# Moving four small SBUF tiles in the allocation order of a fused two-layer feed-forward kernel, and dropping a spare one

## What is computed

```python
# x [2, 4096, 192], weight_gen [2, 4096, 8, 7]; all arrays float32
w = softmax(weight_gen, axis=-1)                       # 7 taps for each of 8 heads
x = einsum('bshk,bskhg->bshg', w, windows_of_7(x))     # causal, zero-padded
g, val = x @ w_gate, x @ w_val                         # 192 -> 1536
x = (g * sigmoid(g) * val) @ w_out                     # 1536 -> 192
h = x @ w_in                                           # 192 -> 2048
out = (h * clip(h + 3, 0, 6) / 6) @ w_out2             # 2048 -> 192
```

## The kernel before

| tensors | bytes each | first start | remainder by 2048 |
|---|---|---|---|
| all weights, `stage`, `taps` | 3072 to 14336 | 16512 | 128, and for `stage1`, `stage3` 1152 |
| `window` | 7680 | 149760 | 256 |
| `sum_even`, `sum_odd`, `prod_even`, `prod_odd` | 3072 | 157440 | 1792, 768, 1792, 768 |
| `conv_main`, `conv_tail` | 2048, 1024 | 169728 | 1792, 1792 |
| `out_tail` | 1024 | 172800 | 768 |
| `half_col`, `warm`, `spare` | 4, 4, 320 | 173824 | 1792, 1824, 1856 |
| `in1_*`, `in2_*` (eight) | 2048 | 174208 | 128 |
| `mid_main`, `mid_tail`, `swapped` | 2048 | 190592 | 128 |
| `hidden`, `hid_hi`, `hid_lo` | 4096, 8192, 8192 | 196736 | 128 |
| `out_main`, `out_other` | 2048, 1024 | 217216 | 128 |
| `out_rows`, `ident` | 3072, 512 | 220288 | 1152, 128 |

## Time and profile before

### The profile page before, as it was taken

One profiled execution on the slowest core, in us unless ns is written; L12 is line 12 of the kernel. 1 busy time (PEld: TensorE's weight loads), 2 busy tenths in 40 slices (PEclk: granted clock), 3 DMA queues, 4 the chain that ended last, 5 costly groups with the idle time before them and its releaser, 6 DMA issues.

```text
span 1269.5 us, 26488 instructions
## 1 busy us (share of the span) xinstructions
PE 1220.7 (96%) x10696; PEld 1032.1 (81%) x10696; DVE 881.0 (69%) x1353; ACT 650.9 (51%) x1178; POOL 57.6 (5%) x43
## 2 busy tenths in 40 slices
PE   5779999999999999999999999999999999999998
PEld 4557888888898888888888888888889888888876
DVE  7688676676867768686776867667686766864554
ACT  1554654546455453645546464554645545364554
POOL 6441100000000000000000000000000000000000
PEclk9899999999999999999999999999999999999999
DMA  5330001001010100101000010100101010000000
GB/s 163 87 112 23 11 1 44 2 1 44 1 45 1 39 7 1 45 1 44 1 22 24 1 44 2 44 1 7 39 2 44 1 44 2 1 13 1 14 13 14
DMA packets 11766, 32.00 MB, mean 25 GB/s; under 512 B 1048, under 2 KB 5784, under 8 KB 11544
## 3 DMA queue, kind: packets, MB, share of 16 engines
q1 hardware_dynamic: 11672, 30.53, 7.4%
HBM read 24.24 MB, written 6.29 MB: 24 GB/s over the span
## 4 chain that ended last, share of the span: by engine, by line
PE 70%; DVE 13%; ACT 11%; issue 3%; DMA 1%; POOL 0%; ACTq 0%; SPq 0%; POOLq 0%
PE up_bank L787 27%; PE acc L802 16%; PE up_bank L793 14%; PE acc L809 11%; DVE hid_lo L672 6%; DVE hidden L667 5%; ACT hidden L431 5%; DVE in_tail_lo L686 2%; ACT hid_hi L438 1%; PE up_bank L1024 1%; ACT in_tail_hi L453 1%; DMA stage<-in_moe_w_gate_dram 1%; DMA stage<-in_moe_w_val_dram 1%; ACT in_hi L450 1%; ACT swapped L461 1%
## 5 line engine op out<-in xcount | busy, mean ns | idle before, releaser
L787 PE MATMUL up_bank<-in_hi,up_hi 64*128 64x512 f32 x1280 | 350.7, 395 | 18.0 <-DVE hidden L664 12.3
L809 PE MATMUL acc<-hid_hi,dn_tail 64*128 64x512 f32 x872 | 342.4, 393 | 11.6 <-DVE hid_lo L672 10.7
L787 PE MATMUL up_bank<-in_hi,up_lo 64*128 64x512 f32 x1280 | 346.2, 388 | 0.0
L787 PE MATMUL up_bank<-in_lo,up_hi 64*128 64x512 f32 x1280 | 345.9, 388 | 0.0
L802 PE MATMUL acc<-hid_hi,dn_hi 64*128 64x512 f32 x872 | 342.3, 393 | 0.0
L802 PE MATMUL acc<-hid_lo,dn_hi 64*128 64x512 f32 x872 | 337.4, 387 | 0.0
L802 PE MATMUL acc<-hid_hi,dn_lo 64*128 64x512 f32 x872 | 337.3, 387 | 0.0
L809 PE MATMUL acc<-hid_lo,dn_tail 64*128 64x512 f32 x872 | 337.3, 387 | 0.0
L667 DVE SCALAR_TENSOR_TENSOR hidden<-hidden,up_bank 128x512 f32<-128x512 f32 x256 | 176.1, 688 | 209.7 <-ACT hidden L431 208.5
L672 DVE TENSOR_TENSOR hid_lo<-hidden,hid_hi 128x512 fp32r<-128x512 f32 x448 | 313.0, 699 | 1.0
L431 ACT ACTIVATE hidden<-up_bank,half_col 128x512 f32<-128x512 f32 x256 | 176.4, 690 | 242.0 <-DVE hid_lo L672 129.7
(11 more groups left out here) (87 smaller groups left out, 1400.1 us busy)
## 6 DMA issues: line engine op xcount, KB each, us to landing
window<-in_x_dram SPq DMA_DIRECT2D x14, 960.0 KB
out_dram<-out_rows SPq DMA_DIRECT2D x16, 384.0 KB, 2.3
stage<-in_moe_w_out_dram SPq DMA_DIRECT2D x7, 384.0 KB, 3.5
window<-in_x_dram SPq DMA_DIRECT2D x4, 472.5 KB
taps<-in_weight_gen_dram SPq DMA_DIRECT2D x1, 1568.0 KB, 13.0
stage<-in_moe_w_in_dram SPq DMA_DIRECT2D x4, 256.0 KB, 2.7
stage<-in_moe_w_gate_dram SPq DMA_DIRECT2D x3, 256.0 KB, 2.7
stage<-in_moe_w_val_dram SPq DMA_DIRECT2D x3, 256.0 KB, 8.3
```

The costliest lines, as they stand in the source:

```text
L787: return nc.tensor.matmul(dst[:, :], w[lane[half], col:col + P], a[lane[half], :], start=first and product == 0, stop=False)
L809: return nc.tensor.matmul(acc[y][1], dn_tail[y][lane[half], k, :], a[lane[half], n % RING, :], start=half == HIGH and product == 0 and k == 0,
```

## The change

The tile `spare` (80 columns, read and written by nothing) is no longer made. `out_tail` is made after `out_main` and no longer before `in1_*`; `half_col` and `warm` are made last. No instruction is added, removed or moved; what differs is addresses.

```diff
         conv_main = sb("conv_main", [P, STEPS, P])
         conv_tail = sb("conv_tail", [P, STEPS, TAIL])
-        out_tail = sb("out_tail", [P, COLS // 2])
-        half_col = sb("half_col", [P, 1])
-        warm = sb("warm", [P, 1])
-        spare = sb("spare", [P, 80])
...
         out_main = sb("out_main", [P, COLS])
 
+        out_tail = sb("out_tail", [P, COLS // 2])
         out_other = sb("out_other", [P, COLS // 2])
         out_rows = sb("out_rows", [P, STEPS * D])
         share_sum = hidden[:, :, :].rearrange("p a c -> p (a c)")[:, 0:STEPS * D]
         share_prod = out_rows[:, :]
         ident = sb("ident", [P, P])
+        half_col = sb("half_col", [P, 1])
+        warm = sb("warm", [P, 1])
```

## The result

| | before | changed |
|---|---|---|
| median of the runs | 1271.57 us (4 runs, 1271.27 to 1272.74) | 1291.54 us (4 runs, 1291.0 to 1292.0) |
| span of the profiled execution | 1269.5 us | 1289.5 us |
| head, up to the first block's copy to `out_rows` | 210.0 us | 211.5 us |
| middle stage | 977.7 us | 995.3 us |
| tail | 81.8 us | 82.7 us |

The ratio is 1.0155, with a 95% interval of 1.0138 to 1.0173: slower by 20 us, far outside the range of the prediction. Moving tiles with no instruction changed costs 1.5%.

What follows compares the result with a forecast made beforehand. TensorE, busy 96% of a 1269.5 us span, was taken to bound the kernel. Five terms of 0 added to the profiled execution's 1271.35 us gave a forecast of 1271.4 us, range 1268.9 to 1273.9.

Steps and rivals of the forecast that it cites:

- No count changes, only durations by place: Whole kernel: no instruction, semaphore or DMA changes, so only durations that depend on where an operand lies can differ.
- VectorE, ScalarE and `half_col` cost nothing: Instructions on moved tiles: 0 us, with bounds of 0.3 us either way for VectorE, -0.5 to +2.0 us for ScalarE.
- "So 0" for TensorE reading moved tiles: TensorE's large moving operands, remainder 128 to 768: 0 us, bounds 2.2 us either way, from equal medians over weight remainders.
- a clash between two engines would show as scatter: TensorE's reads beside other engines' accesses: an address clash would scatter its period time, which repeats to 0.01 us.
- "the same 13.4 ns stand with every weight remainder": Each TensorE slot's 13.4 ns beyond its columns: dependence on present places, 72 us at the far end, excluded from the range.
- "TensorE reads the moved operands at another pace": Rival at TensorE's matmul slots: two cycles per slot, 4.5 us, 1275.8 or 1266.9; chance 0.04 slower, 0.04 faster.
- The prediction's last lines: Layer 1 tiles: 3.18 us or more (or 3.16 or less) with all other medians equal would mean TensorE.
- The first rival's 59 ns and 1291.2 us: Split of next input and tail: moved ring slower for ScalarE or VectorE; 59 ns an instruction is 19.8 us; chance 0.06.
- The store: Last store from `out_rows`, moved by 384 bytes: 0 us, bounds 0 and +2.2 us.
- The estimate of 0.1 us: Last store: rows now starting on a 256-byte boundary save 4 of 100 beats; range and chances stand without it.
- The head: Rival in the head: another order of DVE and POOL meetings or a weight's landing, up to 1 us; within the 0.80.

Runs made afterwards that it cites:

- `e11_sources_only`: Kernel before with `mid_main`, `mid_tail`, `swapped` and `hidden` alone, tiles TensorE never reads, moved to remainder 768 by 2048: 1271.74 us.
- `e12_pairs_alone`: Kernel before with matmuls appended at its end, mostly half-row pairs, at distances of 0 to 512 bytes between weights and moving operand: 1501.53 us in all.

## Why the prediction was wrong

**No count changes, only durations by place:** right. The profile shows the same instructions on each engine.

**VectorE, ScalarE and `half_col` cost nothing:** right; 684 for 685, 610 for 610, 688 for 690 ns, and `e11_sources_only` at 1271.74 us.

**"So 0" for TensorE reading moved tiles:** this is the step that failed. The argument was that weight tiles already go through four remainders with equal medians and an equal pace. But the four remainders, 128, 640, 1152 and 1664, are all 128 by 256, the modulus that counts, and every moving tile was at 128 by 256 as well: four rows that looked like four cases were one. What the runs showed in its place: the distance between the two operands of TensorE sets its pace, 226.7 ns a slot at 0 by 256 bytes and 232.4 at 128. The rows of the transposes did hold two distances (`conv_main` and `out_main` against `ident`), but I compared weight loads, and the weight loads of the up-projections have a median of 184 ns in both kernels (L787, L786): their time does not tell the pace of a stream of 512 columns. The other argument was that a clash between two engines would show as scatter. It says nothing of two reads of TensorE's own: `e12_pairs_alone` shows the effect without another engine, and its unequal slots come in a pattern that repeats, so a period's sum repeats too. Nor was the exclusion of a dependence on place by "the same 13.4 ns stand with every weight remainder" worth anything, for the same reason.

**The size:** the rival "TensorE reads the moved operands at another pace" was the right mechanism, given 4% on the slow side and priced at two cycles, 4.5 us. It is 5.7 ns, nearly 14 cycles of 0.42 ns, as a mean. In full, 5348 x 5.7 = 30 us; 20 were paid. In the middle stage 8635 / 2 slots make 24.6 us against 17.6: 4.4 of the missing 7.0 is idle time that TensorE had before and fills now, most of it around the split of the inputs. In the head and the tail they make 5.9 against 2.4. The remainder is in part the count, which takes in transposes and warm-up matmuls, and otherwise not accounted for. The prediction's last lines did name the sign to look for, a layer 1 tile at 3.18 us or more with all other medians equal; it is 3.254.

**The first rival's 59 ns and 1291.2 us** come within 0.4 us of the result by chance. Its mechanism did not happen.

**The store:** 0, as predicted; the median to landing is 2.3 us in both kernels. The estimate of 0.1 us by the Trainium skill's rule ("DMA: Bandwidth & Descriptors", "How a descriptor splits into AXI transactions") is too small for any run here to show.

**The head:** put at no effect, but 1.5 us of the loss lie there, and TensorE is busy 1.3 us longer in it (179.85 for 178.51). Whether its events kept their order, no view here shows.

## What to carry to other kernels

When a kernel that TensorE paces changes its time although its instructions did not change, compare the distance of matmul starts in a steady stretch, and then the start addresses of weights and moving operand against each other by 256 bytes. Give operands of large fp32r matmuls (512 moving and 128 weight columns; narrower ones gained nothing) starts that agree by 256 bytes on purpose, and not by the sum of what happens to be allocated ahead of them; here a tile that nothing used did it. And before equal rows are taken as proof that something does not matter, ask whether they really differ in the thing that changes.

## What the hardware showed that I had not expected

- In fp32r matmuls of 512 moving and 128 weight columns, one after the other, the pace depends on the distance between the two operands' starts: 227 ns at 0, 256 and 512 bytes, 229 at 64, 231.5 at 16, 232 to 234 at 32, 48, 96, 128, 160, 192 and 224. Half-row pairs and whole-row matmuls behave alike, and other engines have no part in it.
- The place of the operands does not matter while their distance stays: both moved by 640 bytes cost nothing (1271.89 us).
- A slow slot is not slow evenly: at 128 bytes whole-row slots go through 228 to 241 ns in a cycle of seven, at 0 they stay at 226 to 227.
- With 256 moving columns or 64 weight columns the order turns round, by 0.5 to 2 ns, and with 128 moving columns the distance makes no difference.
- Part of the operands at the wrong distance costs nearly as much as all (17.2 of 20 us for the inputs alone), since matmuls on unmoved operands slow down with the others: a layer 1 tile takes the same 3.254 us.
